# Expert blocks of three tiles ahead of those of four, the last block of an expert at 384, 448 or 512 columns, and one table made later

## The reference

```python
# 1: linear attention with decay, 4 batches x 8 heads x 768 steps x 64
state = gamma * state + k[t] outer v[t];  y[t] = scale * q[t] @ state
# 2: each token goes to one of 8 experts
logits = x @ w_gate + modality_bias[modality_id];  e = argmax(logits)
out[e == i] = gate_w * (relu(x[e == i] @ w1[i]) @ w2[i])      # 512 -> 1024 -> 512
# 3: bilinear layer
h = ((x @ w1) * (x @ w2)) @ w3;  return h @ w_out
```

## Time and profile before

| what | value |
| --- | --- |
| median of 3 runs | 833.06 us (831.8 to 833.7) |
| the profiled execution's own time | 832.92 us |
| its span, first to last instruction | 831.2 us |
| mean granted TensorE clock | 0.993 |
| instructions | 14726 |
| attention, to about | 106 us |
| `w3_product` and tables, to | 158.5 us |
| the eight blocks, from 158.5 us to about | 461 us |
| bilinear stage, to | 831.2 us |

### The profile page before, as it was taken

One profiled execution on the slowest core, in us unless ns is written; L12 is line 12 of the kernel. 1 busy time (PEld: TensorE's weight loads), 2 busy tenths in 40 slices (PEclk: granted clock), 3 DMA queues, 4 the chain that ended last, 5 costly groups with the idle time before them and its releaser, 6 DMA issues.

```text
span 831.2 us, 14726 instructions
## 1 busy us (share of the span) xinstructions
PE 813.5 (98%) x5578; PEld 698.6 (84%) x5579; DVE 414.0 (50%) x663; ACT 291.0 (35%) x465; POOL 176.7 (21%) x208
## 2 busy tenths in 40 slices
PE   9999999999999999999999899999999999999996
PEld 8899878888999998888887688888888888888885
DVE  3567778731312234111143987752577742787500
ACT  1234432431222244122243654423455423454210
POOL 2223002202021120201202133311434212433011
PEclk8999999999999999999999999999999999999998
DMA  9999984433030244210223111241111321111011
GB/s 335 316 327 312 305 322 147 151 104 93 11 102 9 92 152 144 83 50 20 81 95 83 38 52 51 67 149 49 53 64 51 107 97 39 63 51 52 13 48 41
DMA packets 51456, 91.88 MB, mean 111 GB/s; under 512 B 8529, under 2 KB 15313, under 8 KB 51409
## 3 DMA queue, kind: packets, MB, share of 16 engines
q1 hardware_dynamic: 41728, 68.47, 24.7%
q0 software_dynamic: 4736, 14.72, 5.5%
q10 hardware_dynamic: 4946, 8.08, 2.7%
HBM read 71.03 MB, written 20.22 MB: 110 GB/s over the span
## 4 chain that ended last, share of the span: by engine, by line
PE 92%; DVE 4%; issue 2%; ACT 0%; POOLq 0%; POOL 0%; DVEq 0%; ACTq 0%
PE bank L470 37%; PE attn L470 33%; PE pair L470 8%; PE bank L998 3%; PE attn L1025 3%; PE pair L1010 3%; PE pair L1103 2%; PE bank L1037 1%; PE attn L1016 1%; PE bank L975 1%; PE bank L1187 1%; DVE w3T L1284 0%; DVE wlo L1284 0%; DVE we_p L1284 0%; PE pair L982 0%
## 5 line engine op out<-in xcount | busy, mean ns | idle before, releaser
L470 PE MATMUL attn<-hT,we_p 128*128 128x512 f32 (+1 forms) x672 | 141.7, 367 | 0.0
L470 PE MATMUL bank<-xT,we_p 128*128 128x512 f32 (+1 forms) x672 | 138.2, 366 | 1.0 <-issue 1.0
L470 PEld LDWEIGHTS bank<-xT,we_p 128*128 128x128 f32 x672 | 122.0, 188 | 16.3 <-issue 1.4
L470 PEld LDWEIGHTS attn<-hT,we_p 128*128 128x128 f32 x672 | 121.2, 188 | 14.4
L470 PE MATMUL attn<-wc,gT 128*128 128x512 f32 x576 | 131.5, 389 | 0.0
L470 PEld LDWEIGHTS attn<-wc,gT 128*128 128x128 f32 x576 | 108.1, 188 | 22.5
L1531 DVE SCALAR_TENSOR_TENSOR hT<-bank,hT 128x512 fp32r<-128x512 f32 x56 | 38.7, 691 | 145.8 <-ACT hT L766 145.8
L470 PE MATMUL bank<-yhi,whi 128*128 128x512 f32 x240 | 93.8, 391 | 2.6 <-DVE wlo L1284 1.9
L470 PE MATMUL bank<-yhi,wlo 128*128 128x512 f32 x240 | 93.4, 389 | 0.0
L766 ACT ACTIVATE hT<-bank 128x512 fp32r<-128x512 f32 x56 | 33.5, 599 | 97.1 <-PE bank L470 97.1
L1284 DVE TENSOR_TENSOR wlo<-w_raw,whi 128x768 fp32r<-128x768 f32 (+1 forms) x72 | 54.7, 790 | 16.2 <-POOL w_raw L667 16.2
(11 more groups left out here) (199 smaller groups left out, 1210.0 us busy)
## 6 DMA issues: line engine op xcount, KB each, us to landing
we_raw<-in_moe_w_dram SPq DMA_DIRECT2D x6, 2048.0 KB, 9.5
w_raw<-in_moe_w_dram SPq DMA_DIRECT2D x40, 256.0 KB, 2.8
yT_sorted<-yout ACTq DMA_DIRECT2D x7, 1024.0 KB, 4.3
qkv<-in_q_t_dram SPq DMA_DIRECT2D x24, 256.0 KB, 3.6
qkv<-in_v_dram SPq DMA_DIRECT2D x24, 256.0 KB, 5.1
x_rows<-x_keep SPq DMA_DIRECT2D x24, 256.0 KB, 3.7
y_loaded<-yT_sorted SPq DMA_DIRECT2D x12, 512.0 KB, 4.8
qkv<-in_k_t_dram SPq DMA_DIRECT2D x23, 256.0 KB, 5.0
```

The lines of the kernel that those rows point to most:

```text
L470: i = pe.matmul(out_, left(a), right(b), start=(first and n == 0), stop=(last and n == 2), **kw)
```

## The change

Three things are changed.

1. The order and cut of blocks. An expert's blocks of three tiles now lead. `left` counts its blocks from the end, so that block boundaries are worked out from the last tile backwards: expert 0 gets 3, 3, 3, 4, expert 3 still 4, 4, 4, expert 5 still 1.
2. The word's low bits no longer hold the tiles but a code: 0 for one tile, 1, 2, 3 for `SIZES` = 384, 448, 512 columns. It is the number of tokens of the block, rounded up to 64 and at least 384. `ENDS` (the sorted row at which an expert ends) is kept for it. By the counts above, the blocks are 384, 384, 384, 448 (415 tokens), 512, 512, 512 (478 tokens) and one tile. PE has three unrolled wide bodies instead of two, nested in two tests; ACT and DVE test the same two cases as before with new limits.
3. `need_tab` is made after `wc_lo(7)` instead of ahead of `s_tab`, with a semaphore of its own (`s_need`), for which SP waits ahead of `need(1)`.

```diff
--- before.py
+++ after.py
@@ -66,6 +66,8 @@
     XCH = 16
     NW = (NI + 3 * E) // GT
     MINW = NT // GT
+    STEP = 64
+    SIZES = tuple(range((GT - 1) * P, BANK + 1, STEP))
     HW = 8
     WARM = 10
     assert H * D == DM and DM == BANK and 2 * D == P and GT == B and FF == 2 * BANK and KF == 2 * B and NI % 2 == 1 and GT < 8 and E <= 8 and NW <= 2 * HW and NG % 2 == 0 and KD == 4
@@ -186,11 +188,12 @@
         place_i = r("place_i", [P, 2, NT], I32)
         tile_of = r("tile_of", [P, NT])
         lane_of = r("lane_of", [P, NT])
-        e_sc = r("e_sc", [P, 12, E])
+        e_sc = r("e_sc", [P, 13, E])
         e_int = r("e_int", [P, 2, E], I32)
         r = region(at_s + 16 * KB)
         w_sc = r("w_sc", [1, 6, NW + 1, E])
-        w_k = r("w_k", [1, 6, NW + 1])
+        w_k = r("w_k", [1, 7, NW + 1])
+        w_int = r("w_int", [1, 2, NW + 1], I32)
         g_sc = r("g_sc", [1, NG, NW + 1])
         run_sc = r("run_sc", [1, E, E])
         run_k = r("run_k", [1, E])
@@ -296,6 +299,7 @@
         s_inv = sem("s_inv")
         s_tmeta = sem("s_tmeta")
         s_tab = sem("s_tab")
+        s_need = sem("s_need")
         s_xst = [sem(f"s_xst{late}") for late in range(2)]
 
         s_wohi = sem("s_wohi")
@@ -579,6 +583,7 @@
                 sp.dma_start(y_loaded[:, B21, :, :], chunks(2 * p, HF)).then_inc(s_yl[B21], 16)
 
             total = sp.value_load(num_tab[0:1, 1:2], min_val=MINW, max_val=NW)
+            sp.wait_ge(s_need, 1)
             stores = need(1)
             w_load(1)
             sp.wait_ge(s_w1lo, nrun * KD)
@@ -875,9 +880,9 @@
 
                 word = word_in(act, held)
                 size = size_in(word)
-                with act.If(size > 1):
+                with act.If(size > 0):
                     wide_hidden()
-                with act.If(size < 2):
+                with act.If(size < 1):
                     one_tile_hidden()
                 coming = word_of(act, w + 1)
                 act.reg_mov(held, coming)
@@ -1125,8 +1130,7 @@
                 i.then_inc(s_yp, 1)
 
             def window(w, total):
-                def wide(tiles):
-                    n = tiles * P
+                def wide(n):
                     for f in range(KF):
                         hidden(w, run, n, f)
                     pe.reg_mov(held, word_of(pe, w + 1))
@@ -1168,12 +1172,15 @@
 
                 word = word_in(pe, held)
                 size, run = size_in(word), run_in(pe, word)
-                with pe.If(size > 3):
-                    wide(4)
-                with pe.If(size < 4):
-                    with pe.If(size > 1):
-                        wide(3)
-                    with pe.If(size < 2):
+                with pe.If(size > 1):
+                    with pe.If(size > 2):
+                        wide(SIZES[2])
+                    with pe.If(size < 3):
+                        wide(SIZES[1])
+                with pe.If(size < 2):
+                    with pe.If(size > 0):
+                        wide(SIZES[0])
+                    with pe.If(size < 1):
                         one_tile()
 
             def first_x():
@@ -1383,7 +1390,7 @@
             flat = lambda a: a[:, :, :].rearrange("p e n -> p (e n)")
             link(dve.tensor_tensor_scan(flat(cumt), sm["segment"], bank[7][:, 0:E * NT], 0.0, ALU.mult, ALU.add))
             row = lambda i: e_sc[:, i, :]
-            COUNT, TILES, CUM, USED, RUN, BASE, RUN1, WINS, PREV, SLACK, LAST, TBASE = range(12)
+            COUNT, TILES, CUM, USED, RUN, BASE, RUN1, WINS, PREV, SLACK, LAST, TBASE, ENDS = range(13)
             scan = lambda dst, src: link(dve.tensor_tensor_scan(dst, sm["ones"][:, 0:E], src, 0.0, ALU.mult, ALU.add))
 
             def whole_tiles(dst, src, unit):
@@ -1428,8 +1435,8 @@
             w3_lo(4)
             wc_lo(2)
 
-            scan(row(BASE), row(COUNT))
-            link(tt(row(BASE), row(BASE), row(COUNT), ALU.subtract))
+            scan(row(ENDS), row(COUNT))
+            link(tt(row(BASE), row(ENDS), row(COUNT), ALU.subtract))
             whole_tiles(row(WINS), row(TILES), GT)
             scan(row(CUM), row(WINS))
             link(tt(row(PREV), row(CUM), row(WINS), ALU.subtract))
@@ -1458,50 +1465,51 @@
             wide = [1, n_tab, E]
             per_e = lambda i: of(i).unsqueeze(1).to_broadcast(wide)
             per_w = sm["widx"][one].unsqueeze(2).to_broadcast(wide)
-            past, mine, first, start, finish, tmp = (w_sc[:, i, :, :] for i in range(6))
+            past, mine, left, start, finish, tmp = (w_sc[:, i, :, :] for i in range(6))
             link(tt(past, per_e(CUM), per_w, ALU.is_le))
             link(tt(mine, per_e(PREV), per_w, ALU.is_le))
             link(tt(mine, mine, past, ALU.subtract))
-            link(tt(first, per_w, per_e(PREV), ALU.subtract))
+            link(tt(left, per_e(CUM), per_w, ALU.subtract))
             wc_lo(3)
             w3_lo(5)
             dve.wait_ge(s_inv, 1)
             dve.tensor_copy(tile_meta[:, :, :].rearrange("p a x -> p (a x)"), bank[0][:, 0:2 * NX]).then_inc(s_tmeta, 1)
-            for dst, up in ((start, 0.0), (finish, 1.0)):
-                link(ts(dst, first, up, 3.0, ALU.add, ALU.mult))
-                link(tt(dst, dst, per_e(SLACK), ALU.add))
-                link(ts(tmp, first, up, 4.0, ALU.add, ALU.mult))
-                link(tt(dst, dst, tmp, ALU.min))
-                link(ts(dst, dst, 0.0, None, ALU.max))
-            link(tt(finish, finish, start, ALU.subtract))
+            link(tt(start, left, per_e(SLACK), ALU.min))
+            link(dve.scalar_tensor_tensor(start, left, 3.0, start, ALU.mult, ALU.add))
+            link(ts(tmp, left, -1.0, None, ALU.add))
+            link(tt(finish, tmp, per_e(SLACK), ALU.min))
+            link(dve.scalar_tensor_tensor(finish, tmp, 3.0, finish, ALU.mult, ALU.add))
+            link(dve.scalar_tensor_tensor(finish, finish, 0.0, start, ALU.max, ALU.subtract))
             link(tt(finish, finish, mine, ALU.mult))
             link(dve.tensor_reduce(w_k[:, 0, :], finish, AX.X, ALU.add))
+            link(dve.scalar_tensor_tensor(start, start, -1.0, per_e(TILES), ALU.mult, ALU.add))
+            link(tt(tmp, per_e(ENDS), mine, ALU.mult))
+            link(dve.tensor_reduce(w_k[:, 6, :], tmp, AX.X, ALU.add))
             wc_lo(4)
             w3_lo(6)
             link(tt(tmp, start, per_e(TBASE), ALU.add))
             link(tt(tmp, tmp, mine, ALU.mult))
             link(dve.tensor_reduce(w_k[:, 5, :], tmp, AX.X, ALU.add))
-            link(ts(start, start, float(P), None, ALU.mult))
-            link(tt(start, start, per_e(BASE), ALU.add))
+            link(dve.scalar_tensor_tensor(start, start, float(P), per_e(BASE), ALU.mult, ALU.add))
             link(tt(start, start, mine, ALU.mult))
             link(dve.tensor_reduce(w_k[:, 1, :], start, AX.X, ALU.add))
+            link(tt(w_k[:, 6, :], w_k[:, 6, :], w_k[:, 1, :], ALU.subtract))
+            link(dve.scalar_tensor_tensor(w_k[:, 6, :], w_k[:, 0, :], -float(P), w_k[:, 6, :], ALU.mult, ALU.min))
+            link(ts(w_int[:, 0, :], w_k[:, 6, :], float(STEP - 1), None, ALU.add))
+            link(ts(w_int[:, 1, :], w_int[:, 0, :], int(np.log2(STEP)), None, ALU.logical_shift_right))
+            link(dve.tensor_copy(w_k[:, 6, :], w_int[:, 1, :]))
+            link(ts(w_k[:, 6, :], w_k[:, 6, :], -float(SIZES[0] // STEP - 1), 1.0, ALU.add, ALU.max))
+            link(dve.scalar_tensor_tensor(w_k[:, 6, :], w_k[:, 0, :], -1.0, w_k[:, 6, :], ALU.is_lt, ALU.mult))
             link(tt(past, past, per_e(USED), ALU.mult))
             link(dve.tensor_reduce(w_k[:, 2, :], past, AX.X, ALU.add))
             link(ts(w_k[:, 2, :], w_k[:, 2, :], e_sc[one, LAST, 0:1], None, ALU.min))
             col = lambda a, c: win_tab[:, a:n_tab, c:c + 1].rearrange("p a b -> p (a b)")
             link(ts(w_k[:, 4, 0:1], w_k[:, 2, 0:1], 0.0, 1.0, ALU.mult, ALU.add))
             link(tt(w_k[:, 4, 1:], w_k[:, 2, 1:], w_k[:, 2, 0:n_tab - 1], ALU.subtract))
-            link(dve.scalar_tensor_tensor(w_k[:, 4, :], w_k[:, 4, :], 8.0, w_k[:, 0, :], ALU.mult, ALU.add))
+            link(dve.scalar_tensor_tensor(w_k[:, 4, :], w_k[:, 4, :], 8.0, w_k[:, 6, :], ALU.mult, ALU.add))
             link(dve.scalar_tensor_tensor(col(0, WORD), w_k[:, 2, :], 16.0, w_k[:, 4, :], ALU.mult, ALU.add))
             link(dve.tensor_copy(col(0, START), w_k[:, 1, :]))
             link(dve.tensor_copy(col(0, TILE), w_k[:, 5, :]))
-            link(ts(w_k[:, 3, :], sm["widx"][one], windows, None, ALU.is_ge))
-            link(ts(w_k[:, 3, :], w_k[:, 3, :], float(NT * P), None, ALU.mult))
-            link(tt(w_k[:, 3, :], w_k[:, 3, :], w_k[:, 1, :], ALU.add))
-            wide = [1, NG, n_tab]
-            link(tt(g_sc[:, :, :], w_k[:, 3, :].unsqueeze(1).to_broadcast(wide), sm["gend"][one].unsqueeze(2).to_broadcast(wide), ALU.is_lt))
-            link(dve.tensor_reduce(need_k[:, :], g_sc[:, :, :], AX.X, ALU.add))
```

(14 more changed lines are left out.)

## The result

| what | before | changed |
| --- | --- | --- |
| executions, us | 833.7, 831.8, 833.06, 831.5 | 839.02, 853.62, 853.21, 840.43 |
| median | 832.43 | 846.82 |
| profiled execution's own time | 832.92 | 839.02 |
| its span | 831.2 | 837.2 |
| mean granted TensorE clock | 0.993 | 0.992 |

The changed kernel is slower. Two of its four executions took 839 to 840 us and two 853 us. That is 840 us, inside the range over all cases (829.0 to 844.5) but above the forecast's own (831.8 to 836), and 6 us above its 833.8 us. "No change" did not hold. The median of all four, 846.8 us, lies outside both ranges. What a longer execution looks like is in the third experiment.

The account below looks back on a forecast made before the run. PE, busy 98% of the span, was taken to bound the kernel. Terms -5.15 - 0.98 + 0.6 + 6.3 = +0.8 us on 832.92, run median 0.14 above, gave 833.8 us; own range 831.8 to 836, all cases 829.0 to 844.5.

Parts of the forecast that it names:

- No change: Whole kernel: forecast of 833.8 us lies within the 0.2% or 1.7 us that a measurement can tell; chance 0.37.
- the wait for code at the head: First block: PE's jump over two bodies waits for its code behind queued data; +6.3 us, bounds +1 and +8.
- the columns' gain: Fourth block: 192 products at 448 columns instead of 512 save 5.15 us, bounds 0 and 10.3.
- The rival of the cheap jump: Loop's head: the first jump's code is read ahead of queued data, costing only 2.45 us; 829.8 us, chance 0.28.
- the old gap: Between first and second block: the 0.98 us issue gap goes, since only the single tile's code is jumped over.
- stall at `hidden(4)`: First block at 384 columns: PE waits once for the second weights' split by ACT and DVE; 0.6 us, 0 to 1.5.
- step (c): Fourth block: first jump to the body for 448, under two pieces behind the head; 0, bounds 0 and +2 us.
- sign of being wrong: PE's gaps: the prediction is wrong if one stands where no code is new, such as on the gathers; no size.
- rival of the loop that doesn't fit: PE's loop needs nine pieces; if not kept, jumps back cost 3.3 us, 10.0 us of gaps; 843.8 us, chance 0.30.
- the moved table: Ahead of the first block: six DVE operations, 1.35 us, fall into 2.03 us of DVE idle time; cost 0.
- the tables: DVE ahead of the first block: net -0.2 us, between -0.4 and +0.3, then gone as code transfer sets the time.
- The rule on code: PE's instruction memory: FIFO of eight 16 KiB blocks, unloaded branch targets wait for a DMA; by it 843.8 us.

Follow-up runs that it names:

- third experiment: Changed kernel with SP's next weight load and POOL's second gather held until the first hidden group is multiplied; five executions 832.24 to 836.35 us, seven 846.67 to 852.92.
- eighth: Changed kernel with PE's bodies ordered 384, 448, 512, single tile, tested so each body's end needs one jump, loop moved by 12 instructions; 895.27 us.
- fourth experiment: Changed kernel with PE's bodies in order of first use (384, 448, 512, single tile) in nested tests; 842.43 us, ratio 1.0129 to the kernel before.
- seventh: Changed kernel with three more idle warming matmuls, 12 PE instructions, ahead of the loop; 843.71 us, ratio 1.0137 to the kernel before.
- ninth experiment: Kernel before's order, blocks of four first, with a third body of 320 columns, bodies tested in a chain, loop moved by 12 instructions; 848.34 us.
- fifth experiment: Kernel before with only the table's move: SP's table made after the product's last split, with its own semaphore; one execution, 833.19 us.

## Why the prediction was right or wrong

**Right: what bounds the kernel, and what the third body and the order do.** PE has 92% of the chain before and after, and the forecast was that the wait for code at the head eats the columns' gain. It does: 5.54 us of gap against 6.3 on record, at 6633 ns where "over 6" was written. But the sum ended at no change, and the kernel became slower; the terms below are what was missing. That it is the queued data which makes 6.6 of 3.4 is shown by the third experiment. The rival of the cheap jump (829.8 us) is out.

**Right: the old gap and the stall.** The gap of 0.98 us went for the reason given, a short jump (243 ns) over the single tile. The stall at `hidden(4)` is 0.8 us against 0.6 (0 to 1.5).

**A size: the columns.** On record 5.15 us from a line between 227 and 173 ns, so 200 ns a product. Measured 4.6 us: the products at 448 columns follow one another every 203 ns (24 in 4.87 us), 3 ns above the line. The Trainium skill ("TensorE: Matmul & The Clock Gate", Back-to-back issue gap) gives, for isolated products, the columns over 2.4 GHz and 2.5 ns; an estimate by it is 189 ns for 448. The trace, where each product has a weight load of its own, gives 14 ns more.

**Failed: step (c), "I take 0, bounds 0 and +2 us".** The jump to the body for 448 took 3682 ns and left 2.22 us. The reason for 0 was that the body begins less than two pieces behind the head and one piece is read ahead. That was reading ahead of straight code; at the fourth block the sequencer had been round the loop through other bodies three times, and the piece was not there. The upper bound was the right answer, a little low.

**Failed: the change was followed only to the first entry of each body.** The prediction has no term for the jump at the end of the fourth block: 4051 ns on L1180, to the loop's end, to which three blocks of 384 had already come without a wait. The prediction's own sign of being wrong, a gap where no code is new, is met here. The reading that fits is that what was read for the jump to 448 pushed out what stood there. The transfers bear it out as a count (33 against 29; 27 with two bodies), but no row says which piece left. So the prediction's rival of the loop that doesn't fit had hold of something: the seven pieces before were read as either kept or not kept as a whole, and the runs show something in between, in which single jumps wait. Whether it is three waits (839 us) or every pass (895 us in the eighth) differed with the order of the bodies, their tests and 12 instructions of offset. It also differs from one execution of a program to the next: in the third experiment seven of twelve took 847 to 853 us.

**Failed: the clock.** After the gaps of 5.54 and 1.87 us PE ran at 1.2 GHz for 3 to 3.4 us. That is 1.6 + 1.9 = 3.5 us, more than half of the miss of 5 us (5.8 against 0.8). The prediction priced a gap by its length. How long the gap was doesn't decide it in these runs. Of eleven gaps between 1.87 and 2.66 us around the blocks eight had a slow stretch behind them and three (2.22, 2.56 and one of 2.32) had none. PE's wait of 1.79 us for DVE had one in the fourth experiment and none in the eighth. All eleven gaps above 5 us had one.

**Hidden by luck: the moved table.** "Cost 0, hidden by PE's first hidden groups" holds in the changed kernel only since the code's gap is there. By itself the move costs PE 0.7 us at the first block, while the row taken as cover was DVE's sequencer at work. On the chain ahead of it the tables gave 0.04 us, where 0.2 were on record.

**Luck in the sum.** The attention stage's end, 2.2 us early, hid as much. With an attention stage as long as in the trace of before the changed kernel's profiled execution would stand at some 841 us.

**The rule on code.** The prediction named the Trainium skill ("Runtime: NRT & Kernel Launch", Instruction fetch mechanics) for a first-in, first-out store of eight blocks. What the runs show, the behaviour between "fits" and "doesn't fit", can be read as such a store, in which what a far jump brings pushes the oldest out, needed or not; no row shows the order in which pieces leave. The same section says that reading ahead is purely sequential; the 3682 ns of the jump to 448 agree, since a body that had been jumped over three times was not at hand. Why 12 instructions matter follows from neither sentence.

**What stays open.** Which piece is pushed out at which jump; why the changed kernel takes 839 in one execution and 853 in the next; and why the eighth experiment, with the same bodies in another order, reads its code anew in every pass. A model by which one piece less would fit was behind the expectations of the seventh to ninth experiment, and all three speak against it.

## What to carry to other kernels

A specialised body has a price in code, to be set against what it saves. Here 64 columns in one block brought 4.6 us, and the third body cost 6.0 us with the order as it is, and 5.9 us as dead code in another place. Look at which body the first pass enters, and count the jumps in series that each body's end goes through. Moving the first body to the head took the head's gap away (fourth and eighth experiment), but both kernels were slower in the end, so each order has to be measured. In the profile, "issue" in the chain with no partner, the sequencer's compare-and-branch rows above 3 us and the count of instruction transfers belong together; look at them before and after any change that adds unrolled code, and take several executions, since with this kernel the time isn't fixed.

## What the runs showed of the hardware

- A taken branch to code that isn't at hand held PE's sequencer for 3.3 to 4.4 us in 23 cases (3300 to 4367 ns), with one instruction transfer in each, and for 6.3 to 6.8 us at the loop's head, where the data load just issued fills the DMA engines (four cases, 6283 to 6838 ns; share 0.87 to 0.92). The engine lost the jump's length less the sequencer's lead, 1.1 to 2.6 us where a gap had one long jump.
- Eleven more jumps took 4.5 to 6.6 us away from the head. Each has two instruction transfers in it that start within 0.6 us of one another, as the 6614 ns of the fourth experiment; the DMA share was 0.04 in one of 4532 ns and 1.00 in the jump back of 6303 ns. A piece read ahead behind the jump before may share the queue with the piece waited for; that was not tried.
- Code that no block enters cost 5.9 us.
- A gap of 1.87 us cost 3.8: the granted clock was 0.50 for 3.4 us behind it, which took another 1.9.
- Idle time ahead of a loop's first operation on DVE (2.03 us) was not cover: the sequencer's loop set-up and register reads filled it (159.98 to 162.5 us in the fifth experiment), operations put ahead pushed them back, and the idle time was 2.63 us then.
- Products in this kernel follow one another every 146 ns at 320 columns, 173 at 384, 203 at 448 and 227 at 512.
